# A fused attention, gated layer and expert layer on one core: turned sinks in a bank of their own, the split of x a step later, and four smaller edits

## The reference

```python
# attention: 2 x 8 heads, 768 positions, 64 wide, n_sink = 4, window = 128
keep = is_sink | in_window            # a row sees 4 first keys and its last 128
a = softmax(where(keep, q @ k.T / 8, -1e9)); x = a @ v     # -> x: 1536 x 512
# gated layer: 512 -> 1536 -> 512
y = ((x @ w_a) * (x @ w_b)) @ w_out
# experts: 8 of 512 -> 1024 -> 512, 192 tokens each
logits = y @ w_gate
# all (token, expert) pairs, best first: a token takes the expert if it has
# none yet and the expert has fewer than 192
out[mask_e] = relu(y[mask_e] @ w1[e]) @ w2[e]
```

## Time and profile before

| | us |
|---|---|
| median of 3 runs | 677.68 (677.47 to 682.88) |
| the profiled execution: its time | 678.51 |
| its span in the profile | 676.80 |
| PE busy (matmuls) | 635.9, 94% |
| DVE, ACT, POOL busy | 317.0, 259.0, 315.5 |

### The profile page before, as it was taken

The page is one execution under the profiler, slowest core; times in us unless marked ns, Lnnn a source line. Parts: engine busy times, 40 slices in busy tenths (PEclk is TensorE's granted clock), DMA queues, the critical chain, the costliest instruction groups (busy, mean ns, idle before and its releaser), DMA issues.

```text
span 676.8 us, 12794 instructions
## 1 busy us (share of the span) xinstructions
PE 635.9 (94%) x4692; PEld 527.9 (78%) x4692; DVE 317.0 (47%) x1086; ACT 259.0 (38%) x632; POOL 315.5 (47%) x223
## 2 busy tenths in 40 slices
PE   7888888889999999999999999999959999999995
PEld 5555555689989989998997777777758898888884
DVE  4666665511112332671688998888801111112110
ACT  5677666533332323322341232422234424334330
POOL 7444333545545455454444655000064567655561
PEclk9999998999999999999999999999979999999998
DMA  8253221224445436345413233311468567666500
GB/s 272 84 202 128 72 73 55 63 64 125 125 128 185 125 100 213 99 120 166 147 33 110 77 103 118 141 48 47 152 207 310 203 249 287 259 224 210 203 24 24
DMA packets 76093, 94.34 MB, mean 139 GB/s; under 512 B 4448, under 2 KB 54144, under 8 KB 75392
## 3 DMA queue, kind: packets, MB, share of 16 engines
q1 hardware_dynamic: 73696, 86.82, 38.4%
q0 software_dynamic: 2048, 6.29, 3.0%
q10 hardware_dynamic: 288, 0.41, 0.2%
HBM read 87.16 MB, written 6.34 MB: 138 GB/s over the span
## 4 chain that ended last, share of the span: by engine, by line
PE 76%; issue 10%; POOL 8%; DVE 3%; ACT 1%; DMA 1%; POOLq 0%; DVEq 0%; ACTq 0%
PE bank L1194 14%; PE bank L1075 13%; PE bank L1284 13%; PE bank L1077 12%; PE bank L1076 12%; POOL pn_sb L493 6%; PE bank L1296 4%; PE bank L1087 2%; PE bank L1149 1%; PE bank L1233 1%; PE bank L1269 1%; PE bank L983 1%; POOL wl_ab L483 1%; DVE yhl L906 1%; DMA y_rows<-y_sb 0%
## 5 line engine op out<-in xcount | busy, mean ns | idle before, releaser
L483 POOL TENSOR_TENSOR wl_ab<-raw_ab,wh_ab 128x1024 fp32r<-128x1024 f32 x48 | 114.7, 2391 | 113.2 <-ACT wh_ab L585 113.2
L1075 PE MATMUL bank<-xh,wh_ab 128*128 128x384 f32 x384 | 133.2, 347 | 2.1 <-POOL wl_ab L483 2.1
L1077 PE MATMUL bank<-xh,wl_ab 128*128 128x384 f32 x384 | 128.8, 335 | 0.0
L1076 PE MATMUL bank<-xl,wh_ab 128*128 128x384 f32 x384 | 128.6, 335 | 0.0
L547 POOL TENSOR_TENSOR w2l<-w_raw,w2h 128x1024 fp32r<-128x1024 f32 x32 | 75.1, 2375 | 47.7 <-ACT w2h L692 47.6
L1284 PE MATMUL bank<-xgT,w_sb 128*128 128x192 f32 x512 | 89.2, 334 | 0.9 <-DVE xgT L955 0.9
L1284 PEld LDWEIGHTS bank<-xgT,w_sb 128*128 128x128 f32 x512 | 86.1, 195 | 2.0 <-issue 1.0
L830 DVE TENSOR_TENSOR hid<-hid,bank 128x384 f32<-128x384 f32 x48 | 26.6, 554 | 123.1 <-ACT hid L636 123.0
L493 POOL TENSOR_SCALAR pn_sb<-pe_sb,inv 128x260 f32<-128x260 f32 (+2 forms) x48 | 50.1, 1044 | 68.8 <-DVE inv L776 68.8
L1075 PEld LDWEIGHTS bank<-xh,wh_ab 128*128 128x128 f32 x384 | 72.0, 188 | 12.6 <-issue 9.3
L636 ACT ACTIVATE hid<-bank 128x384 f32<-128x384 f32 x48 | 23.6, 492 | 150.5 <-PE bank L1077 150.5
(11 more groups left out here) (140 smaller groups left out, 1013.2 us busy)
## 6 DMA issues: line engine op xcount, KB each, us to landing
w_sb<-in_moe_w_dram SPq DMA_DIRECT2D x8, 2048.0 KB, 7.9
w_raw<-in_moe_w_dram SPq DMA_DIRECT2D x32, 512.0 KB, 6.8
raw_ab<-in_moe_w_a_dram SPq DMA_DIRECT2D x48, 256.0 KB, 3.0
raw_ab<-in_moe_w_b_dram SPq DMA_DIRECT2D x48, 256.0 KB, 3.3
raw_out<-in_moe_w_out_dram SPq DMA_DIRECT2D x24, 256.0 KB, 2.7
lb<-logit_rows SPq DMA_DIRECT2D x4, 1536.0 KB, 6.5
v_sb<-in_v_dram SPq DMA_DIRECT2D x8, 384.0 KB
woT<-in_moe_w_outT_dram SPq DMA_DIRECT2D x1, 3072.0 KB, 11.4
```

Of the source, the lines that this page charges most:

```text
L483: pool.tensor_tensor(wl_ab[s % 2][:, :], raw_ab[s % 3][:, :], wh_ab[s % 2][:, :].bitcast(F32), ALU.subtract).then_inc(abl_done, 1)
L1075: pe.matmul(dst, lh, rh, start=first, stop=False)
L1076: pe.matmul(dst, lh, rl, start=False, stop=False)
L1077: return pe.matmul(dst, ll, rh, start=False, stop=last)
```

## The change

1. The sink turn goes to bank 7, at one place for all tiles, and waits for the copy of the one before (`sinkT_out`) and for the gate's copy out of that bank. `turn` waits for `xl_done` no more; `values` still does. The gate's steps are one later, its columns go where the turned sinks were, and its rows wait for a sink copy.
2. `x_high` and `x_low` are made a step later (tile g - 5 in step g); ACT makes its part at the step's start, DVE after the masks. The loops of ACT and DVE have 53 steps for 52.
3. The first transfer of q and k covers two tiles for three; 14 identity transposes for 24 stand at the start.
4. The twelve logit products of each of the first three chunks are issued together.
5. The last y block goes tile by tile, three parts each, as the first one already does, for part by part.
6. After the routing 12 identity transposes, and 28 more after `y_stored`, for 20. The gather has a semaphore for each half (`FIRST`, `REST`), and PE waits for them one by one.
7. In the last expert `out_first` comes before `out_rest`, its scatters likewise, and ACT takes one half of the copy of the 64 rows from DVE.

```diff
-    GATE_AT = [DUOS - QT * (NF // FB - i) + 1 for i in range(NF // FB)]
+    FIRST_TILES = 2
+    GATE_AT = [DUOS - QT * (NF // FB - i) + 2 for i in range(NF // FB)]
...
+    def by_tile(z):
+        return z in (0, Y_STEPS - 1)
     def window_of_h(z):
-        return last_window(3 * TY * z + 2 * TY)
+        return last_window(3 * TY * z + (2 if by_tile(z) else 2 * TY))
...
-            for g in range(DUOS + 4):
+            for g in range(DUOS + 5):
+                if g >= 5:
+                    x_high(g - 5)
                 if g < DUOS:
...
-                if g >= 4:
-                    x_high(g - 4)
-
...
-            for g in range(DUOS + 4):
+            for g in range(DUOS + 5):
                 if g < DUOS:
                     mask(2 * g)
                     mask(2 * g + 1)
+                if g - 3 in GATE_AT:
+                    wog_copy(GATE_AT.index(g - 3))
+                if g >= 5:
+                    x_low(g - 5)
...
-                    dve.tensor_copy(sinkT_sb[d % 2][0:2 * n_sink, :], OB_[d % 2][0:2 * n_sink, P:2 * P]).then_inc(sinkT_out, 1)
-                if g - 2 in GATE_AT:
-                    wog_copy(GATE_AT.index(g - 2))
-                if g - 4 >= 0:
-                    x_low(g - 4)
+                    dve.tensor_copy(sinkT_sb[d % 2][0:2 * n_sink, :], TB[0:2 * n_sink, 0:P]).then_inc(sinkT_out, 1)
...
-            keep_clock_up(PT_[0], 24)
+            keep_clock_up(PT_[0], 14)
...
                 if g >= 2:
                     pe.wait_ge(pT_out, g - 1)
-                    pe.wait_ge(xl_done, g - 1)
                 if ns:
-                    pe.transpose(OB_[g % 2][0:2 * ns, P:2 * P], src[:, P:P + ns, :].rearrange("p k h -> p (k h)"),
+                    pe.wait_ge(sinkT_out, sinks_before(g))
+                    turned = sum(at < g + 3 for at in GATE_AT)
+                    if turned:
+                        pe.wait_ge(gateT_out, turned)
+                    pe.transpose(TB[0:2 * ns, 0:P], src[:, P:P + ns, :].rearrange("p k h -> p (k h)"),
                                  ident[:, :])
...
             def gate_rows(i):
+                pe.wait_ge(sinkT_out, sinks_before(GATE_AT[i] - 2))
...
-                if f % FG != FG - 1:
+                each = FG if c == NC - 1 else NF
+                if f % each != each - 1:
                     return
...
-                    part, t = (at % 3, at // 3) if z == 0 else divmod(at, TY)
+                    part, t = (at % 3, at // 3) if by_tile(z) else divmod(at, TY)
...
-            keep_clock_up(banks[7], 20)
+            keep_clock_up(banks[7], 12)
+            pe.wait_ge(y_stored, 16 * NT)
+            keep_clock_up(banks[7], 28)
...
-                pe.wait_ge(yg_in[e % 2], 32 * (e // 2 + 1))
...
                 for h, rows in enumerate((slice(0, FIRST), slice(0, REST))):
+                    pe.wait_ge(yg_in[e % 2][h], 16 * (e // 2 + 1))
...
+                if e + 1 < E:
+                    out_rest(e)
+                    out_first(e)
+                else:
+                    out_first(e)
+                    out_rest(e)
```

More of the change, by code:

```diff
@@ L285, in build @@
         w2h_done, w2l_done = sem("w2h_done"), sem("w2l_done")
-        yg_in = [sem(f"yg_in{i}") for i in range(2)]
+        yg_in = [[sem(f"yg_in{i}{h}") for h in ("first", "rest")] for i in range(2)]
         xg_ready, xg_outA, xg_outV = sem("xg_ready"), sem("xg_outA"), sem("xg_outV")
@@ L352, in load_w1 @@
                     sp.wait_ge(y_stored, 16 * NT)
-                    sp.wait_ge(yg_in[0], 32)
-                    sp.wait_ge(yg_in[1], 32)
+                    for h in range(2):
+                        sp.wait_ge(yg_in[0][h], 16)
+                        sp.wait_ge(yg_in[1][h], 16)
                 if e >= 2:
@@ L531, in gather @@
                         in_offset=bass.IndirectOffsetOnAxis(ap=idx[rows, h, e:e + 1], axis=0)
-                    ).then_inc(yg_in[e % 2], 16)
+                    ).then_inc(yg_in[e % 2][h], 16)
             def scatter(e):
-                for h, rows, copied, copies in ((1, slice(0, REST), rest_out, 2), (0, slice(0, FIRST), o_out, 1)):
+                halves = [(1, slice(0, REST), rest_out, 2), (0, slice(0, FIRST), o_out, 1)]
+                for h, rows, copied, copies in halves if e + 1 < E else halves[::-1]:
                     pool.wait_ge(copied, copies * (e + 1))
@@ L719, in _ @@
                 act.activation(o_sb[e % 2][:, 0, :], O2_[0][:, :], ACT.Copy).then_inc(o_out, 1)
+            act.wait_ge(rest_ready, E)
+            act.activation(o_sb[(E - 1) % 2][0:REST, 1, DM // 2:DM], O2_[1][REST:2 * REST, 0:DM // 2],
+                           ACT.Copy).then_inc(rest_out, 1)
         @block.vector
@@ L972, in _ @@
                     dve.wait_ge(o_stored[e % 2], 32 * (e // 2))
-                for n in range(2):
+                for n in range(2 if e + 1 < E else 1):
                     dve.tensor_copy(o_sb[e % 2][0:REST, 1, n * DM // 2:(n + 1) * DM // 2],
@@ L991, in scores @@
                 rows = slice(D * h, D * (h + 1))
-                if p == 0 and i < QT // 2:
+                if p == 0 and i < FIRST_TILES:
                     pe.wait_ge(q_first, 16)
@@ L1139, in logit_part @@
                 c, f = s // NF, s % NF
-                if f % FG != FG - 1:
+                each = FG if c == NC - 1 else NF
+                if f % each != each - 1:
                     return
                 pe.wait_ge(hm_done, s + 1)
-                if s == FG - 1:
+                if c == 0:
                     pe.wait_ge(wog_done, NF // FB)
-                if f == FG - 1 and c >= 2:
+                if f == each - 1 and c >= 2:
                     pe.wait_ge(LT_out, c - 1)
-                for j in range(FG):
-                    i = f - FG + 1 + j
+                for i in range(f - each + 1, f + 1):
+                    j = i % FG
                     mm = pe.matmul(LT_[c % 2][j * TILE:(j + 1) * TILE, 0:C], wog[:, i, :], hid[:, i, C * c:C * (c + 1)],
-                                   start=(f == FG - 1), stop=(f == NF - 1), skip_group_check=True)
+                                   start=(i < FG), stop=(i >= NF - FG), skip_group_check=True)
                 if f == NF - 1:
```

14 lines of the change are left out of this document (8 added, 6 removed).

## The result

The changed kernel takes 655.57 us (median of 4 runs, 652.96 to 657.99), the kernel before beside it 677.9 (4 runs, 677.47 to 682.88): ratio 0.9654, 95% interval 0.9587 to 0.972. On another chip it took 658.14 (6 runs, 656.02 to 659.63) for 678.62: 0.970, interval 0.9677 to 0.9723. The forecast was 652, with bounds of its own of 648 to 657 and a range of 646 to 662; the median on the other chip lies in the range but outside those bounds.

The account below looks back on a forecast made before the run. Waits in a ring bound attention, PE's own work most of what follows; 18.1 (attention, start, transition) + 1.0 + 1.8 + 4.3 + 0.3 = 25.5 us off the 676.80 span gave 651.3, so 652 as median, range 646 to 662.

Parts of the forecast that it names:

- Attention: Pairs of heads before the gated layer: 12.0 us for 14.48 each, 17.4 us in all (13 to 20).
- The change takes x out of the ring: Attention: turn, values, x_high, x_low, turn set the pace at 2.41 us a step; the turn would need no x_low.
- my balance of the three engines' step: Attention step without waits: PE 2.13 us, DVE 1.92, ACT 1.74, so PE is the fullest.
- The start: Fewer transposes and a smaller first transfer bring tile 3's turn, at 17.36, about 3.0 us earlier (1 to 4).
- The third rival: Start: with 14 transposes the clock doesn't rise, PE bounds attention at 1.2 GHz, up to 703 us; chance 0.04.
- the rival's "against": Third rival, attention of before: the clock fell once and rose again within some 3 us by attention's own work.
- Transition: Attention to gated layer: PE arrives earlier and waits for POOL about 2.0 us for 0.28, a loss of 1.8 (0.3 to 2.5).
- Logits and y: Gated layer and last y block: six bursts fewer save 1.0 us (0 to 1.4), y by tiles 1.8 (1.4 to 2.2).
- the halves: Gather before the first expert: four of eight transposes done before its last rows, 1.25 us less.
- 3.03 less if the clock stays up: First expert: 56 records in 9.10 us for 12.13, if the handover's transposes keep the clock up.
- The second rival: Handover: transposes don't hold the clock, 5.2 us lost, 657.4 us; chance 0.12.
- The tail: Last expert's end: ACT and DVE copy 64 rows together and the last scatter is half as long, 0.3 us (0 to 0.8).

Follow-up runs that it names:

- the bank alone: The changed kernel with the split of x back at its old place, sink turns still in bank 7: 668.33 us, ratio 0.9835 to the kernel before.
- attention alone: Only items 1 and 2 of the change, all else as in the kernel before: 663.72 us, ratio 0.9782 to the kernel before.
- the nine starts above: Nine profiles of kernels with 14 identity transposes at the start: tile 3's sink turn at 14.21 to 17.69 us, mean 16.04.
- weights early, products at the handover: The changed kernel with gate weights' splits earlier and identity products for the handover's transposes: 652.06 us, ratio 0.9613; changed kernel beside it 658.14 us.

## Why the prediction was right, point by point

**Attention.** A pair at 12.0 us and a wait of 0.4 for the sink copy: 12.02 and 0.33. The stage up to the first gated product gave 15.3 us for 15.1. From the sink turn of one pair's fourth tile (i = 3) to that of the next it was 14.48, 14.48, 14.48, 14.74, 16.54, 16.58 and 18.02 us, and is now 12.01, 12.02, 12.02, 12.01, 14.72, 14.72 and 15.59 (the last three hold the gate's steps, the last one of before also its low stretch). The gate's rows do wait now, 0.44 us each for the 0.67 that I had taken:

```profile
70.68 1.07 PE L1047 MATMUL bank<-woT,wg 128*32 128x512 f32 x8 [0.44 <-DVE sinkT_sb L798]
```

The mechanism was half of it. "The change takes x out of the ring" named one ring, over PE's turn; the bank alone showed that this is worth 0.40 us of the 2.46 and that ACT and DVE had a second one of the same length. The forecast came out because the change opened both, and because my balance of the three engines' step was right: PE is the fullest.

**The start.** 3.0 us were forecast. In three profiles it is 2.8 to 3.15, in the profiled execution 0.98, and in the worst the turn comes 0.3 later than before. The third rival had the right mechanism, a clock that doesn't rise with 14 transposes, and the wrong length: the slow start ends between 13.7 and 17.5 us and costs up to 3.5 us, since attention's own work raises the clock, as the rival's "against" says.

**Transition.** Forecast a loss of 1.8, measured 1.8: the last pair takes 0.87 us more than the two before it, and from the last pair's turn to the first gated product it is 2.75 for 1.83. The waits themselves are longer than foreseen (3.0 in two pieces for 2.0). Not foreseen at all: the clock falls there. 6.8 us at 0.50, from 111.1 to 117.9, cost 2.5 us in the profile (363.75 for some 361.3). This is the largest miss, and the prediction had no term for it.

**Logits and y.** 1.7 us for 1.0 and 2.5 for 1.8: both above the upper bound I gave (1.4 and 2.2). For the logits I had priced start and drain of a burst at 0.2; at 1.7 for six bursts it is 0.28. Of the y term the copies are as forecast (they end 1.38 us earlier against the list, for 1.45), and the gather starts 2.42 us earlier against it: stores and gather gave 1.04 where I allowed nothing to 0.7.

**The handover.** The step "with 12 + 28 transposes PE works until about y_stored + 3.4 us" held, the wait of 6.02 is gone and the halves gave their 1.25. "3.03 less if the clock stays up" did not: 1.16. (With the clock up it would have been 2.79, 9.34 for 12.13; the 9.10 that I subtracted is from another view.) The second rival, with its chance of 0.12, is what happened here, at 1.9 us for the 5.2 it had named, since the transposes ran at full rate first and the clock fell only at 483.2.

**The tail.** 0.3 us as forecast: from PE's last product to the end of the span it is 6.48 for 6.79.

The Trainium skill's rule ("TensorE: Matmul & The Clock Gate", Part 4), that transposes don't count as work for the clock, is borne out at the handover in so far as the clock fell in seven of eight profiles with 40 of them. Two things speak against it: with none the clock fell sooner and for longer (478.3 to 488.5), and the start. Timeline of attention alone, where PE has done nothing but transposes:

```profile
1.58 1.75 PE L989 MATMUL bank<-ident 128*128 128x128 f32 x7 [1.58 <-POOL ident L436]
...
4.63 1.15 PE L989 MATMUL bank<-ident 128*128 128x128 f32 x9
```

250 ns each at first and 128 later: they raised their own clock. So the rule as it stands is too strong for this kernel, and what transposes lack at the handover that products have stays open. The Trainium skill also says, in Part 1 of the same page ("What's actually happening"), that the count of slow matmuls at a kernel's start differs from run to run; the nine starts above, 14.2 to 17.7 us behind the same 14 transposes, agree.

**The sum.** Forecast span 651.3, profile 655.9. Missing are 2.0 at the start, 2.5 in the gated layer and 1.9 at the first expert, nearly all of it clock; more than forecast are logits 0.7, y 0.7, attention 0.2 and the experts 0.2. The two executions with a mean clock of 0.996 had 651.2 and 651.4. That they meet the 651.3 is luck in part: larger gains from logits and y stand against clock that was still lost, and with every stretch but one avoided (weights early, products at the handover) the span was 649.7.

## What to carry to other kernels

When a step waits in a ring, count the rings: list for each engine what stands behind the waiting instruction, and sum each closed path; two of the same length look like one. When a change makes a tuned kernel denser, forecast with the clock's price as a range of its own, because slow stretches can stand behind gaps of 1 to 2 us at a stage's seam, in some executions and not in others. Products, not transposes, over one gap and work moved out of another gave 6 us here together, of which the profiles account for 4.8; each by itself could not be told from nothing in the total.

## What the runs showed of the hardware

- What a stretch at 0.50 costs: 6.8 us of it in the gated layer 2.5 (and 3.0 in two pieces), 3.4 us at the first expert 1.6 (10.97 for 9.34). At the expert that is nearly half its length, in the gated layer about 0.4 of it.
- The granted clock's record read 1.00 for up to 12 us at the start in which PE's transposes took 0.28 us instead of 0.16 (four profiles with 14 transposes, one with products). At the start of a trace the durations are the better witness.
- Beside POOL's split of the weights (2.35 us) a DVE operation on 128 x 2 elements took 1.50 us, in the kernel before 2.03; away from it 0.16. Timeline after:

```profile
109.82 2.35 POOL L489 TENSOR_TENSOR wl_ab<-raw_ab,wh_ab 128x1024 fp32r<-128x1024 f32 x1
...
110.69 1.50 DVE L786 TENSOR_SCALAR rowsum_eps<-rowsum 128x2 f32<-128x2 f32 x1
```

It ended at 112.19, POOL's at 112.17; in the kernel before both ended at 128.5. In the three profiles in which POOL's split was moved away, none of the 48 such operations took more than 0.28 us. So it is one of the reasons why the last tiles come late in the transition; how much of the 1.33 us it is, no run separates.
